# Dummy matrix products ahead of TensorE's waits in the head of a fused attention and MLP kernel, and one normalisation moved ahead of GpSimd's sums of v

## The reference, cut to what matters

```python
# attention: q, k, v are (4, 8, 576, 64); factor = 4; scale = 1/8
q_d, k_d, v_d = (t.reshape(B, H, 144, 4, 64).mean(axis=3) for t in (q, k, v))
out_up = np.repeat(sm_attn(q_d, k_d, v_d), 4, axis=2)          # pooled attention
mask = np.abs(pos[:, None] - pos[None, :]) < 4
out_local = softmax(np.where(mask, scale * q @ k.T, -1e9)) @ v  # band of 7 keys
x = (out_up + out_local) as (2304, 512)
y = ((x @ w_a) * (x @ w_b)) @ w_out                             # 512 -> 1536 -> 512
h = y @ w_in; solu = h * softmax(h)                             # 512 -> 1024
out = layernorm(solu) * g_ln @ w_out2                           # 1024 -> 512
```

## Time and profile before

| | |
|---|---|
| median of 3 runs | 786.36 us (786.12 to 787.45) |
| the profiled execution | 787.3 us, its span 785.5 us |
| PE busy | 760.1 us (97%) |
| DVE busy | 559.7 us (71%) |
| ACT busy | 298.4 us (38%) |
| POOL busy | 211.2 us (27%) |
| mean granted clock | 0.993 |

### The profile page before, as it was taken

How to read it: one execution, slowest core, us unless ns; L and a number is a source line. 1 busy time by engine, 2 the same in 40 slices (tenths; PEclk the granted TensorE clock), 3 DMA queues, 4 the chain that set the end, 5 groups by cost and what they waited for, 6 DMA issues and landing times.

```text
span 785.5 us, 12293 instructions
## 1 busy us (share of the span) xinstructions
PE 760.1 (97%) x4440; PEld 699.4 (89%) x4440; DVE 559.7 (71%) x977; ACT 298.4 (38%) x819; POOL 211.2 (27%) x264
## 2 busy tenths in 40 slices
PE   6999999898999999999999999999999999999998
PEld 5778899798999999998999999999988888888886
DVE  4589999979868987778777876122467767666663
ACT  3544747263353535353424424234322212222222
POOL 3468898355423330051001111122100000000000
PEclk9999999999999999999999999999999999999999
DMA  9999846586788575582755433536121011011011
GB/s 185 216 226 229 199 119 198 153 260 186 228 206 228 145 206 172 161 221 70 215 146 169 135 106 111 194 115 215 54 67 51 30 55 52 29 55 51 30 41 41
DMA packets 86573, 109.41 MB, mean 139 GB/s; under 512 B 20081, under 2 KB 53361, under 8 KB 86513
## 3 DMA queue, kind: packets, MB, share of 16 engines
q1 hardware_dynamic: 71792, 99.12, 46.9%
q10 hardware_dynamic: 14721, 9.51, 4.3%
HBM read 87.76 MB, written 20.84 MB: 138 GB/s over the span
## 4 chain that ended last, share of the span: by engine, by line
PE 77%; POOL 2%; DMA 1%; issue 0%; ACT 0%; SPq 0%
PE psum L872 24%; PE psum L874 24%; PE psum L873 24%; PE psum L985 2%; PE psum L829 1%; POOL raw L1723 1%; DMA raw<-in_q 1%; PE psum L809 1%; PE psum L840 1%; PE psum L819 1%; POOL raw L1727 1%; PE psum L791 0%; ACT out_sb L1283 0%; ACT out_d L1099 0%; SPq L510 0%
## 5 line engine op out<-in xcount | busy, mean ns | idle before, releaser
L872 PE MATMUL psum<-x_hi,w_hi 128*128 128x384 f32 x576 | 199.3, 346 | 2.6 <-POOL w_lo L1735 1.6
L874 PE MATMUL psum<-x_hi,w_lo 128*128 128x384 f32 x576 | 194.2, 337 | 0.0
L873 PE MATMUL psum<-x_lo,w_hi 128*128 128x384 f32 x576 | 194.1, 337 | 0.0
L872 PEld LDWEIGHTS psum<-x_hi,w_hi 128*128 128x128 f32 x576 | 109.3, 190 | 6.9 <-issue 3.7
L873 PEld LDWEIGHTS psum<-x_lo,w_hi 128*128 128x128 f32 x576 | 109.3, 190 | 0.0
L874 PEld LDWEIGHTS psum<-x_hi,w_lo 128*128 128x128 f32 x576 | 109.1, 189 | 0.0
L1411 DVE TENSOR_TENSOR ab_f<-psum,a_sb 128x384 f32<-128x384 f32 x72 | 39.9, 554 | 93.5 <-PE psum L874 63.2
L872 PE MATMUL psum<-ab_hi,wo_hi 128*128 128x384 f32 x288 | 101.4, 352 | 3.4 <-issue 3.4
L874 PE MATMUL psum<-ab_hi,wo_lo 128*128 128x384 f32 x288 | 98.2, 341 | 0.0
L873 PE MATMUL psum<-ab_lo,wo_hi 128*128 128x384 f32 x288 | 98.1, 341 | 0.0
L1723 POOL TENSOR_TENSOR raw<-raw 96x256 f32<-96x256 f32 x60 | 56.2, 962 | 120.1 <-DMA raw<-in_q 54.6
(11 more groups left out here) (148 smaller groups left out, 1422.9 us busy)
## 6 DMA issues: line engine op xcount, KB each, us to landing
wo_hi<-wo_hi_scratch SPq DMA_DIRECT2D x53, 256.0 KB, 2.7
wo_lo<-wo_lo_scratch SPq DMA_DIRECT2D x53, 256.0 KB, 3.2
wo_raw<-in_moe_w_out SPq DMA_DIRECT2D x19, 256.0 KB, 4.3
raw<-in_v SPq DMA_DIRECT2D x8, 576.0 KB, 7.7
yT_scratch<-y_sb ACTq DMA_DIRECT2D x6, 768.0 KB, 6.5
y_raw<-yT_scratch SPq DMA_DIRECT2D x18, 256.0 KB, 3.0
out<-out_sb SPq DMA_DIRECT2D x18, 256.0 KB, 2.1
k_u<-in_k SPq DMA_DIRECT2D x11, 384.0 KB
```

The costliest lines, as they stand in the source:

```text
L872: mm(dst, wh, xh, start=first, stop=False, skip_group_check=not check)
L873: mm(dst, wh, xl, start=False, stop=False, skip_group_check=not check)
L874: last = mm(dst, wl, xh, start=False, stop=end, skip_group_check=not check)
```

## The change

TensorE gets a helper, `keep_busy(n, count)`, that issues `count` products of 128 x 128 by 128 x 128 in `f32`, both operands from `xup`, into bank `n`, where nothing of use stands at that time. Thirteen calls with 47 products in all are put into the head's order. VectorE fills the two slices of `xup` with 1.0 as its first instruction. Four waits are named ahead of such calls, which the real instructions behind them have in any case. On GpSimd `normalise(2)` goes from behind the sums of v of batch 0 to ahead of them.

```diff
+            def keep_busy(n, count):
+                for _ in range(count):
+                    mm(bank(n, 128), xup[:, 0, :], xup[:, 1, :], start=True, stop=True)
...
                 last.then_inc(s.h_turned, 1)
+                if c == 0:
+                    keep_busy(5, 3)
                 at_least(pe, s.kd_ready, c)
...
+            pe.wait_ge(s.ones_ready, 1)
+            keep_busy(5, 6)
             pe.wait_ge(s.ident_ready, 1)
             head_turn(0)
+            keep_busy(5, 2)
             head_scores(0)
             head_turn(1)
+            keep_busy(5, 2)
             head_scores(1)
             head_turn(2)
+            keep_busy(5, 4)
             head_turn_p(0)
             head_scores(2)
+            keep_busy(5, 3)
             head_values(0)
             head_turn(3)
             head_turn_p(1)
             head_scores(3)
+            pe.wait_ge(s.x_local, 1)
+            keep_busy(5, 2)
             head_values(1)
             head_pooled_scores(0)
             head_pooled_scores(1)
             head_turn_p(2)
+            pe.wait_ge(s.x_local, 2)
+            keep_busy(5, 5)
             head_values(2)
+            keep_busy(3, 2)
             head_pooled_scores(2)
             head_pooled_scores(3)
             head_turn_pooled(0)
             head_turn_p(3)
+            pe.wait_ge(s.x_local, 3)
+            keep_busy(5, 2)
             head_turn_pooled(1)
+            keep_busy(5, 5)
             head_values(3)
+            pe.wait_ge(s.h_masked, PPB)
+            keep_busy(2, 8)
             head_up(0)
...
             head_up(3)
+            keep_busy(GA, 3)
             up_product(0, 0, WA)
...
+            V.memset(xup[:, 0:2, :], 1.0).then_inc(s.ones_ready, 1)
             head_qT(0)
...
             normalise(0)
             normalise(1)
+            normalise(2)
             pool_rows(0, 2, 0)
             pool_rows(0, 2, 1)
-            normalise(2)
             normalise(3)
```

More of the change, by code:

```diff
@@ L382, in build_program @@
         y_loaded1 out_stored0 out_stored1
-        act_begun ident_step ident_ready edge_ready band_ready pads_ready
+        act_begun ones_ready ident_step ident_ready edge_ready band_ready pads_ready
         h_turned qT_by_vector qT_by_scalar kT_ready kd_ready qd_summed qd_ready h_scored h_masked h_exped h_inv_ready h_normed h_p_turned h_pT_ready h_x_mm
```

## The result

The changed kernel takes 790.28 us (median of 5 runs, 789.11 to 792.20), the kernel before beside it 786.36 (785.58 to 787.45). The ratio is 1.0052, with a 95% interval of 1.0033 to 1.0071: half a per cent slower, 3.9 us by the medians, where 1.1 us was forecast. The profiled execution is the fastest of the five (789.11), and its span of 787.3 us is only 1.8 above. So the two traces serve for places and times, and the size of the loss comes from the ratios.

What follows compares the result with a forecast made beforehand. VectorE sets the pace from about 60 us, so only its gates' delay counts: span 785.5 + 1.1 = 786.6 us, 788.4 with 1.8 around it, 787.5 against the median, as the profiled execution lies 0.94 above; range 783.5 to 793.5.

Steps and rivals of the forecast that it cites:

- rival B: TensorE's clock rises late, at the eight dummies before `head_up(0)` or thereabouts; 792 us, from 789 to 795; chance 0.27.
- the chain over SP: GpSimd's late sums of v delay SP's stores, the `v_d` load, `raw<-in_q` and w_lo(2); the last three by 2.0 us.
- The dummies' price: On TensorE, each dummy is two records and costs 0.47 us at the low clock level, about 0.25 at the high.
- the filled `xup` costs nothing: VectorE's fill of `xup` lies ahead of its first work and costs nothing; uncovered, under 0.54 us.
- The level: TensorE's clock in the head is high early; its own 33 us of work there shrink to about 18.
- When the inverse comes: The third inverse, which GpSimd's moved `normalise(2)` waits for, ends at 25.2 us instead of 29.3; sums of v 4.0 late.
- The 2.7 us: TensorE from 18.88 us to the fourth pair's turn of k takes 4.6 us, with three dummies, instead of 7.3.
- The 1.4 us: Saved ahead of 18.88 us: two groups of scores save 1.0 each, loads of q and k give some back.
- What of it gets through: Of 4.0 us delay in the sums of v, SP's `v_d` load is 1.5 to 3.9 late; 2.0 taken.
- w_lo(2), with its stall and the lost clock, sets gate(2): Block 2's product ends at 74.3 us, 2.0 late plus 1.8 of lost clock; VectorE's `gate(2)` follows at 74.4, 1.1 late.

Runs made afterwards that it cites:

- sums held: Kernel before, no dummies, old order; GpSimd's sums of v of batch 1 wait for VectorE's first `x_lo`: 789.45 us, 1.0050.
- w_lo(2) early: GpSimd's `weight_low(2)` put between the two halves of the sums of q: on the kernel before 785.44 us, 0.9995; on the changed kernel 789.28 us, 1.0051.
- more dummies: Changed kernel with 14 more dummies, in the turns of the second and third pair and ahead of the fourth turn of p: 788.38 us, 1.0036.
- dummies in the stall: All dummies, `normalise(2)` in its old place, and 16 more dummies in TensorE's wait ahead of block 2, against the kernel before: 785.83 us, 1.0016.

## Why the prediction came out as it did

**The time: inside the range, and in part by the range's width.** 790.28 us lies in the 783.5 to 793.5 of the prediction, and in the forecast's own 785.2 to 791, but also in rival B's 789 to 795. The forecast had the way right (slower) and 1.1 us where 3.9 were measured.

**That the move costs, and the chain over SP: right as far as it was tested.** The move is the cause: alone, with no dummy in it, it has a ratio of 1.0051, and the dummies without it 1.0009. In the five kernels with the move ahead of both halves each link of the chain that the prediction read is late, from the sums of v over the stores, the load of `v_d` and `raw<-in_q` to GpSimd's w_lo. How the loss gets from there to VectorE is argued and not shown. For GpSimd's queue, and against the late `v_d` itself, speak "sums held", in which `v_d` is on time (34.80) and the loss is there, and the table. But with the move VectorE is late at `gate(0)` too, and no kernel has the move with only one of the two.

**The dummies' price: right.** 0.47 and 0.25 us were forecast, two records each; 0.49 and 0.25 were measured. So was "the filled `xup` costs nothing".

**The level: in part.** The forecast had it high early and kept; rival B had it rise late and fall in the turns. It rose at 6.4, fell at 13.3, came back at 20.1 and was low again from 37.1 to 40.5. I had read the low level of the kernel before as what the head's own work does, and that was wrong: it was one execution. In the kernel before with w_lo(2) early, whose head is the same, the turn of p and the scores change level without one dummy:

```profile
18.85 1.50 PE L726 MATMUL psum<-ident,p_loc 128*70 128x128 f32 x6 [0.32 <-POOL p_loc L1715]
20.28 2.28 PE L716 MATMUL psum<-kT,qT 64*128 64x70 f32 x24
...
24.38 0.82 PE L726 MATMUL psum<-ident,p_loc 128*70 128x128 f32 x6
25.32 1.29 PE L716 MATMUL psum<-kT,qT 64*128 64x70 f32 x24
```

The records put the rise at 22.5 us there. So little of the gain that I gave to the dummies was theirs to give. The Trainium skill, page "TensorE: Matmul & The Clock Gate", Part 4: PE-mode transpose, says that transposes don't engage the high level; in this trace the rise comes among scores, behind turns, so it can't tell. The kernel with more dummies kept the level from 13.3 us on through its turns, with dummies between them.

**When the inverse comes: mis-sized.** The term was 29.3 - 2.7 - 1.4 = 25.2 us. It came at 28.08 + 0.19 = 28.3, and even with the level held high at 27.38 + 0.19 = 27.6. The 2.7 us were there: from the first turn of p to the inverse 7.7 us, 10.4 before. The 1.4 us ahead of it were not: that turn started at 20.55 us, 1.7 later than before (18.88), behind a wait of 2.18 us for k and six dummies at the low level. The sums of v came 6.8 late instead of 4.0.

**What of it gets through: inside the range, at the wrong end.** The range for `v_d` was 36.1 to 38.5, and I took 2.0 us of delay from its low end; it was 3.6. The stores were issued 6.8 us late and the load 3.6, so the empty DMA queues gave back 3.2, as argued. The product of block 2, forecast at 67.4, started at 68.44, as GpSimd came to w_lo(2) 3.0 us late instead of 2.0; the stall was 4.2 us instead of 7, because TensorE came to it only at 64.2, the window behind was at 0.50 as forecast, and the product ended at 75.0 for 74.3. `gate(2)`, forecast at 74.4, came at 75.64.

**Where the step failed: "w_lo(2), with its stall and the lost clock, sets gate(2)".** The prediction added the stall and the clock to the end of the product and let `gate(2)` follow 0.1 us behind. In its own rows the product ended at 70.5 and the gate came at 73.31, and VectorE has no wait between its first subtraction and `gate(2)`, before or after. The kernel with w_lo(2) early has no such stall and is as slow (1.0051), and the one with a high clock behind the stall is no faster. So 74.4 for 75.64 is near the mark partly by luck. What the traces show in its place is a VectorE that is busy throughout: it came to `gate(0)` 2.15 us late, and one of its instructions is held for most of GpSimd's burst, which ends 3.7 us later than before; the gate follows that end by 2.4 us at the least. Which of the two sets `gate(2)` in the change is open. The Trainium skill, "SBUF — State Buffer", Who interferes with whom, has the shared port locked exclusively; the rows agree that the cost moves from one instruction to another (5.21, 5.89, or 2.92 and 3.35 us) and doesn't go away.

**Two things were not in the sum.** `normalise(3)` stands behind the sums and was 2.75 us late (36.12, before 33.37), which TensorE felt as a wait of 1.72 us; by the kernel with dummies in the stall, whose head ends as late and which loses 0.16%, the late end of the head alone isn't the loss. And behind `gate(2)` a further 0.9 us is lost until `gate(6)` (35.6 us for 34.7); what makes it isn't shown. From `gate(6)` on the traces run parallel, 3.2 us apart, until the clock of the kernel before falls at 185 us and takes back 1.5. The forecast's 1.1 us against 3.9 is thus a sum of sizes: 1.2 more at `gate(2)`, 0.9 behind it, and the rest lies between one execution and the medians.

**What stays open.** No kernel was made in which only `raw<-in_q` is late, so its delay is not priced by itself, nor one with the move in which VectorE comes to `gate(0)` on time. "Sums held" loses as much as the move with a smaller delay at `gate(2)`; its 4.7 us of waits behind that gate say where, but not why TensorE and ScalarE come late there.

## What to carry to other kernels

Before you move an instruction ahead of others in an in-order queue, write down when its operand is ready and what every instruction behind it, and each DMA behind those, loses: here 0.9 us of work that had to wait for 5.7 cost half a per cent. An engine that looks far from the bound (GpSimd, 27% busy) can still cost time if its bursts hold up instructions of the full engine. Before you let one event follow another in a forecast, look whether the later one waited for the earlier: `gate(2)` waited for its product in neither kernel. The dummy products raised the clock in the head and gained nothing here, where VectorE is the full engine behind it, and a clock level read from one execution is no property of the kernel.

## What the runs showed of the hardware

- The same dummies raise the level at quite different times: the first record of 1.00 stands at 6.4 us in the change, at 4.6 to 5.1 in three other kernels with this head, and at 20.8 and 22.0 in two more; with 14 more dummies it stands at 13.3. Without dummies it came from 22.5 to 27.6 in four kernels and at 35.1, 54.6 and 55.3 in three.
- One VectorE instruction can be held through several of GpSimd's instructions, not only the one that it met: a TENSOR_SCALAR of 128 x 2, 0.16 us elsewhere, took 5.2 us, and a product of 128 x 768, 0.94 elsewhere, 5.9, each through most of a burst of eight subtractions.
- A TensorE that is never idle can stay at 1.2 GHz for 6.5 us, and 16 dummies in a stall kept it at 2.4 GHz behind it, where the same kernel without them had 0.50 for 10.2 us.
